# The two first-layer sets of a token-tile pair become one, ahead of the pair's first product

## What is computed

```python
for _ in range(8):                      # gates: 8 rounds of row and column scaling
    P /= P.sum(1, keepdims=True) + 1e-09
    P /= P.sum(0, keepdims=True) + 1e-09
    P *= N / E
for e in range(E):                      # E = 8, w1[e] 512 x 1024, w2[e] 1024 x 512
    h = np.maximum(x @ w1[e], 0.0)
    ye = h @ w2[e]
    out += P[:, e:e + 1] * ye
```

## Time and profile before

| | |
|---|---|
| Runs | 1045.05 us median of 3 (1040.86 to 1045.7) |
| Profiled execution | 1040.46 us, its span 1038.4 us |
| TensorE matmuls | busy 1005.9 us (97%), 8667 matmuls |
| VectorE | busy 755.6 us (73%) |
| ScalarE | busy 583.1 us (56%) |
| GpSimd | busy 609.5 us (59%) |
| Mean granted TensorE clock | 0.988 of full |

### The profile page before, as it was taken

How to read it: one execution, slowest core, us unless ns; L and a number is a source line. 1 busy time by engine, 2 the same in 40 slices (tenths; PEclk the granted TensorE clock), 3 DMA queues, 4 the chain that set the end, 5 groups by cost and what they waited for, 6 DMA issues and landing times.

```text
span 1038.4 us, 25583 instructions
## 1 busy us (share of the span) xinstructions
PE 1005.9 (97%) x8667; PEld 926.5 (89%) x8667; DVE 755.6 (73%) x2042; ACT 583.1 (56%) x1368; POOL 609.5 (59%) x520
## 2 busy tenths in 40 slices
PE   8999988999989999999999999999999999999998
PEld 5787753469989999999989999999899999999998
DVE  6877742537898778777767788688668777878685
ACT  6677731244558656645664665465546564755552
POOL 5454530014586749666965697578647874977543
PEclk9999988989999999999999999999999999999999
DMA  5677248930200220022002200400130022000111
GB/s 186 228 269 285 73 163 339 408 143 2 82 2 1 83 82 2 2 83 83 2 4 86 79 2 2 156 8 1 52 116 1 2 81 84 2 2 22 62 41 62
DMA packets 36903, 87.79 MB, mean 85 GB/s; under 512 B 2976, under 2 KB 2976, under 8 KB 36768
## 3 DMA queue, kind: packets, MB, share of 16 engines
q1 hardware_dynamic: 36768, 86.07, 22.8%
HBM read 81.35 MB, written 4.72 MB: 83 GB/s over the span
## 4 chain that ended last, share of the span: by engine, by line
PE 60%; POOL 17%; issue 14%; DVE 5%; ACT 2%; DMA 1%; POOLq 0%; ACTq 0%; DVEq 0%
PE bank L783 13%; PE bank L785 12%; PE bank L787 12%; POOL s_split L491 11%; PE bank L733 4%; PE bank L560 3%; PE bank L570 3%; POOL t_split L496 3%; PE bank L589 3%; PE bank L670 2%; PE bank L607 1%; DMA mid_raw<-slot_w_in 1%; PE bank L677 1%; PE bank L711 1%; PE bank L601 1%
## 5 line engine op out<-in xcount | busy, mean ns | idle before, releaser
L491 POOL TENSOR_TENSOR s_split<-s_sum,s_split 128x512 fp32r<-128x512 f32 x288 | 372.1, 1309 | 322.2 <-ACT s_split L896 317.5
L1265 DVE SCALAR_TENSOR_TENSOR acc<-bank,gate_now,acc 128x256 f32<-128x256 f32 x441 | 227.1, 516 | 137.8 <-PE bank L787 136.5
L896 ACT ACTIVATE s_split<-s_sum 128x512 fp32r<-128x512 f32 x288 | 181.6, 632 | 248.5 <-PE bank L787 127.7
L783 PE MATMUL bank<-t_split,s_split 128*128 128x256 f32 x1008 | 283.4, 281 | 2.9 <-DVE acc L1265 1.7
L785 PE MATMUL bank<-t_split,s_split 128*128 128x256 f32 x1008 | 281.3, 279 | 0.0
L787 PE MATMUL bank<-t_split,s_split 128*128 128x256 f32 x1008 | 281.2, 279 | 0.0
L783 PEld LDWEIGHTS bank<-t_split,s_split 128*128 128x128 f32 x1008 | 191.3, 190 | 7.6 <-issue 5.7
L787 PEld LDWEIGHTS bank<-t_split,s_split 128*128 128x128 f32 x1008 | 189.5, 188 | 0.0
L785 PEld LDWEIGHTS bank<-t_split,s_split 128*128 128x128 f32 x1008 | 189.3, 188 | 0.0
L783 PE MATMUL bank<-t_split,a 128*128 128x256 f32 x576 | 162.1, 281 | 5.3 <-DVE acc L1259 2.7
L785 PE MATMUL bank<-t_split,a 128*128 128x256 f32 x576 | 160.5, 279 | 0.0
(11 more groups left out here) (171 smaller groups left out, 1973.7 us busy)
## 6 DMA issues: line engine op xcount, KB each, us to landing
raw<-big_w_in SPq DMA_DIRECT2D x15, 2048.0 KB, 8.7
slot_raw<-slot_w_in SPq DMA_DIRECT2D x14, 1024.0 KB, 6.7
mid_raw<-slot_w_in SPq DMA_DIRECT2D x6, 1024.0 KB, 10.1
early_raw<-slot_w_in SPq DMA_DIRECT2D x6, 1024.0 KB, 11.0
late_raw<-slot_w_in SPq DMA_DIRECT2D x6, 1024.0 KB, 8.3
q_ring<-q_tiles SPq DMA_DIRECT2D x18, 256.0 KB, 5.1
k_ring<-k_tiles SPq DMA_DIRECT2D x18, 256.0 KB, 5.3
v_ring<-v_rows SPq DMA_DIRECT2D x18, 256.0 KB, 2.7
```

Source lines behind the costliest of these rows:

```text
L491: pool.tensor_tensor(s_split[:, i, 1, :, :], s_sum[:, i, :, :], s_split[:, i, 0, :, :].bitcast(F32), ALU.subtract)\
L783: pe.matmul(to, left[:, 0, f, :], t_place(parity, k, 0)[:, f, :], start=(f == 0 and k in FRESH), stop=False, skip_group_check=k not in FRESH)
L896: act.activation(s_split[:, i, 0, :, :], s_sum[:, i, :, :], ACT.Copy).then_inc(s_hi_ready, 1)
L1265: done = dve.scalar_tensor_tensor(out=to, in0=got, scalar=gate, in1=to, op0=ALU.mult, op1=ALU.add)
```

## The change

TensorE issues both sets of the next pair's first layer in a row, ahead of product 0, instead of the first ahead of product 0 and the second ahead of product 2. The waits and signals inside `hidden` are the same. No other engine's program is changed.

```diff
                     e1, p1, parity1, n1, before = next_pair(e, p, parity, first)
                     for k in range(PRODUCTS):
                         if ahead and k == 0:
-                            hidden(e1, p1, parity1, 0, n1, before)
-                        if ahead and k == 2:
-                            hidden(e1, p1, parity1, 1, n1, before)
+                            for s in range(2):
+                                hidden(e1, p1, parity1, s, n1, before)
                         if not last and (p, k) == (G_TILE_PAIR, 3):
                             pe.wait_ge(g_lo_ready, GROUPS * e + GROUPS)
                             g_products(e + 1)
```

## The result

The changed kernel takes **1036.63 us** (median of 6 runs, 1034.42 to 1037.33) beside 1043.2 us for the kernel before (median of 6, 1040.86 to 1045.7): a ratio of 0.9942, 95% interval 0.9925 to 0.9959. The mechanism that came true is that of the second rival, "the pace locks fast" (chance 0.20). That its figure, 1036.6 us, is also the measured one is luck: it was counted from a median of three runs, 1045.05 us, that six runs put at 1043.2, its stalls were too small and its pace gain took an all-fast pair for 10.47 us where it takes 10.51.

The account below looks back on a forecast made before the run. TensorE, busy 97% of the span, was taken as the bound. Stalls of 0.6 + 1.9 + 0.4 = +2.9 us and a pace term of 0, on a median of 1045.05, gave 1048.0 us, range 1038 to 1057.

Parts of the forecast that it names:

- the second rival: TensorE's products: a set of eight leaves them all at the fast pace, net -8.5 us, 1036.6 us; chance 0.20.
- the one on the pace: Undisturbed pairs on TensorE: the two matmul paces, 113.3 and 117.8 ns, even out, so this term is taken as 0.
- The upper bound of +1.4: Upper bound kept for the pace term, which was itself taken as 0; the lower bound was -2.7 us.
- some eight matmuls after a set begins: Point for the pace locking fast: the slow pace is left about there today, and a set of eight has them inside.
- it leaves the fast pace at once too: Argument against the pace locking fast: behind a first-layer set TensorE also goes from fast to slow at once.
- The stalls: TensorE's waits at the start, at expert boundaries and in gate rounds, summed to +2.9 us.
- start of the first pair: At 230 us the moved set waits for VectorE's very first sums, with products 0 and 1 queued behind: +0.6 us, once.
- product 4 behind four expert ends: At 445, 646, 848 and 947 us GpSimd's gapless queue shifts by 0.47, so each stall grows: 4 x 0.47 = +1.9 us.
- product 3 at 345 us: Stall at 343 us for VectorE, which waits for ScalarE's accumulator scaling, the end of a shifted ScalarE queue: +0.4 us.
- gate rounds of the first expert: Three stalls, 3.9 us, at 292, 309.60 and 317: the moved set fills or gives back each 0.47 shift, net 0.
- Cost nil: Back edges at 540 and 740 us: TensorE waits before product 3 for VectorE, whose resumption the shift does not touch; 0.
- the slack before product 4: Ordinary pairs: product 4 has 1.8 us of slack behind addition 1, 1.4 afterwards, so the 0.47 shift costs nothing.
- ScalarE's earlier copies: ScalarE's copies of half s = 1 no longer wait 1.07 us for TensorE; worth nothing, as VectorE never waited for them.

Follow-up runs that it names:

- sets_at_0_and_1: Against the kernel before: two sets of four first-layer matmuls, ahead of products 0 and 1 instead of 0 and 2; 1043.21 us, ratio 1.0008.
- t4_on_vector: Against the changed kernel: VectorE computes T4's low part in place of B22's, and GpSimd takes B22's; 1035.55 us, ratio 0.9941.
- all_three: Changed kernel with T4's and B22's low parts swapped between engines, `g_products` ahead of the set of eight, odd experts' T4 part behind addition 0; 1035.01 us, ratio 0.9939.

## Why the prediction was wrong

**The step that failed** is the one on the pace: "I take 0 for this term, since both patterns end near it and only a one-sided lock would not, and keep -2.7 and +1.4 as its bounds." The lock is one-sided. In undisturbed pairs the kernels with eight ahead of product 0, with eight ahead of product 1 and with two sets of eight all have the fast pace behind the run, whichever came before it; in `sets_at_0_and_1` two separate sets of four bring each pair back to the pace it began with. The term is -9.5 us over the 47 undisturbed pairs, where the second rival had -11.4, and -10.8 in experts 1 to 7 with their disturbed pairs. The upper bound of +1.4 comes out of no sum that the prediction shows. The reason for the lock also stood in the prediction, "some eight matmuls after a set begins" the slow pace is left, but the argument against it ("it leaves the fast pace at once too") took a set of eight for a set of four followed by four more of the same effect. The length enters by a beat, and no row of before, with its fours only, could have told eight from nine. What rows could have told is that the bounds weren't bounds: three outcomes (flip, lock fast, lock slow) were named, and the zero was chosen from the one in the middle.

By the Trainium skill ("TensorE: Matmul & The Clock Gate", Back-to-back issue gap) an isolated gap at 256 columns is 109.2 ns, as an estimate from that page; the formula has no term for what went before, and the page gives it for a single matmul, not for a stream with weight loads. In this stream the same matmuls took 113.4 or 117.8 ns, by what ran ahead of them, at a granted clock of 1.00 both times. So the formula gave no ground for a term of 0.

Two more terms belong to the way from 1048.0 to 1036.63. The forecast was counted from 1045.05 us, the median of three runs; from the 1043.2 of six it would be 1046.1. In the other direction, a drop of the granted clock in expert 0, which the prediction had no term for, cost the profiled execution some 1.5 us.

**The stalls** were forecast at +2.9 us and are +5.7:

```
                                     forecast   measured
start of the first pair               +0.6      +0.72
product 4 behind four expert ends     +1.9      +3.14   (0.58, 0.77, 0.57, 0.62 -> 1.40, 1.41, 1.41, 1.46)
product 3 at 345 us                   +0.4      +0.79
product 3 behind two back edges        0        +1.55   (0.75, 0.67 -> 1.44, 1.53)
gate rounds of the first expert        0        -0.7    (3.9 -> 3.2)
L733 at the two back edges             0        +0.2
```

- The mechanism at product 4 is the forecast one: the queue of GpSimd hangs on the end of product 0 of the pair before and has no gap. The size is off because the shift isn't 0.47 alone. TensorE also arrives earlier, since it now goes through the products between at the faster pace. Before, at 445, 848 and 947 us, products 2 to 6 of the last pair and 2 and 3 of the new one were slow, 84 matmuls, now 4.4 ns shorter each: 0.37 us. 0.47 + 0.37 = 0.84; the three stalls grew by 0.82, 0.84 and 0.84. At 646 us the last pair had been fast already, and only products 0, 1 and half of 2 of the new one were slow: 30 x 4.4 ns = 0.13, and 0.60 in all; that stall grew by 0.64. So the trace itself separates the two parts. A gain in pace turns into a stall wherever another engine sets the time.
- "Cost nil" at the back edges was wrong. The reason given was that VectorE resumes "after a time that the shift does not touch". It does resume about when it did (4.97 us after the last addition, was 4.65), but then its B22 part runs into GpSimd's T4 part. GpSimd and VectorE at the first back edge, in the changed kernel:

```profile
541.29 2.40 POOL L496 TENSOR_TENSOR t_split<-raw,t_split 128x1024 fp32r<-128x1024 f32 x1
...
542.68 2.09 DVE L1110 TENSOR_TENSOR t_split<-raw,t_split 128x1024 fp32r<-128x1024 f32 x1 [4.97 <-issue]
```

and at the second one, in the kernel before:

```profile
741.91 2.40 POOL L496 TENSOR_TENSOR t_split<-raw,t_split 128x1024 fp32r<-128x1024 f32 x1
...
744.14 1.26 DVE L1111 TENSOR_TENSOR t_split<-raw,t_split 128x1024 fp32r<-128x1024 f32 x1 [5.05 <-ACT t_split L905]
```

  VectorE's instruction ends at 544.77, GpSimd's at 543.69: 1.08 us apart; before, 745.40 and 744.31: 1.09. The experiments' kernels have 1.08 to 1.09 at the same place, but for one meeting of 0.01 us. So VectorE's end hangs on GpSimd's end, GpSimd's on the same shifted queue, and the stall before product 3 grows as that before product 4 does: 0.69 and 0.86. The prediction had both rows side by side and used the overlap for the three `sum_lo` only. The Trainium skill ("SBUF — State Buffer", Who interferes with whom) calls the port pair that the two engines share "an exclusive lock" and says that issue order decides who blocks. By that rule the end would be fixed by GpSimd's end; the trace agrees: 1.08 us of the instruction lie behind that end, and with GpSimd idle all of it takes 1.22 (at 202.94 us).
- The stall at 345 us grew by the 0.4 forecast and as much again (0.79): there too products 2 to 6 of the last pair had been slow.

**Right** were: the 0.6 us at the start (0.72, with the releaser named); no wait of the moved set for the sums in any other pair; ordinary pairs without a gap in TensorE, the slack before product 4 taking the 0.47; ScalarE's earlier copies worth nothing; VectorE's 0.38 us unchanged; the first expert's stalls at about nothing (-0.7; its half-clock stretch was not foreseen); GpSimd's and VectorE's overlap in the `sum_lo` unchanged (4.78).

**Open.** Why first-layer matmuls have the beat of five, and why the products settle at two paces, no run shows; that they do, and which lengths leave which pace, is shown for 2, 4, 6, 8, 9, 10 and 12 in this stream only, with one trace of each kernel. Why the edits to the stalls don't add up in `all_three` is open as well, and so is what brings a half-clock stretch behind one idle gap and not behind another.

## What to carry to other kernels

Where an engine is busy 97% of the span, count the distance of its instruction starts, group by group, before touching their order: here it had two values 4% apart, and how many matmuls of another kind stood in a row chose between them. If a term is unknown and its outcomes are discrete, give the outcomes and measure the cheapest kernel that tells them apart; the middle is not an estimate. And when one engine gets faster, each stall whose end another engine sets grows by what was gained since that engine's last dependence on it.

## What was unexpected in the hardware

- Matmuls of 128x128 by 128x256 ran at 113.4 or 117.8 ns from start to start at an unchanged granted clock. From the fast pace, runs of 2, 6, 8, 10 and 12 first-layer matmuls left it fast, runs of 4 and 9 slow. From the slow pace, runs of 4, 8, 9, 10 and 12 ended it, and a run of 6 ended it behind `g_products` and behind one stall, but not behind another; the 16 `g_products` ahead of product 3 left the slow pace behind them in the changed kernel. The whole is worth 9.5 us in the 47 undisturbed pairs, 0.9% of this kernel.
- Inside such a run, begun at the fast pace, the distances repeat with period five: 122, 120, 119, 115, 118 ns.
- The granted clock fell to 0.50 for 3.4 us at a time, once or twice behind the 229 us in 12 of the 16 traces, each time at the end of an idle gap of TensorE, at a gate round or a back edge, or up to 1.6 us behind it (the gaps were 1.76 to 3.15 us long); other such gaps, as the 2.15 us at 291.95 in the kernel before, were followed by none. In expert 0 of the changed kernel it cost some 1.5 us, and at the back edge of `t4_on_vector` next to nothing, since a stall behind it vanished.
- A VectorE instruction with two SBUF inputs (128x1024) that met a GpSimd one under way ended 1.08 to 1.09 us behind it in 31 of the 32 meetings at the back edges of the 16 traces, and took 1.26 to 2.64 us accordingly (in the 32nd it began 0.01 us before GpSimd's end and took its usual 1.22); three GpSimd instructions take 3.76 us alone and 4.8 with VectorE's among them.
- Around the loop's back edge VectorE stood still for 4.45 to 5.07 us and TensorE for 1.55 to 2.28 ahead of its first instruction, in all 16 traces; no edit tried here took a clear part of it.
